# Pooling of the two kv batches: the first by image row and a matmul, the second in short GpSimd additions

## What is computed

```python
def _attn_ref(q, kv, w_sr):            # q (2, 12288, 128), kv (2, 384, 32, 128)
    kv_pool = kv.reshape(B, H // 4, 4, W // 4, 4, C).mean(axis=(2, 4))
    kv_flat = kv_pool.reshape(B, -1, C) @ w_sr        # 768 keys of each batch
    k = v = kv_flat
    s = scale * (q @ k.transpose(0, 2, 1))
    s = s - s.max(-1, keepdims=True)
    a = np.exp(s)
    a /= a.sum(-1, keepdims=True) + 1e-09
    return a @ v
x = attn_out.reshape(24576, 128)
h = x @ moe_w_in;   x = (h * np.cos(h)) @ moe_w_out              # 128 -> 2048 -> 128
h = x @ moe2_w_in;  out = (h / (1 + np.exp(-1.702 * h))) @ moe2_w_out
```

## Time and profile before

| | us |
|---|---|
| median of 3 runs | 2780.97 |
| lowest, highest | 2780.66, 2782.22 |
| span of the profiled execution | 2781.5 |
| PE busy in it | 2704.7 (97%) |
| DVE, ACT, POOL busy | 2056.6, 2151.9, 1152.9 |

### The profile page before, as it was taken

One profiled execution on the slowest core, in us unless ns is written; L12 is line 12 of the kernel. 1 busy time (PEld: TensorE's weight loads), 2 busy tenths in 40 slices (PEclk: granted clock), 3 DMA queues, 4 the chain that ended last, 5 costly groups with the idle time before them and its releaser, 6 DMA issues.

```text
span 2781.5 us, 40487 instructions
## 1 busy us (share of the span) xinstructions
PE 2704.7 (97%) x13112; PEld 2220.0 (80%) x13112; DVE 2056.6 (74%) x2852; ACT 2151.9 (77%) x2673; POOL 1152.9 (41%) x622
## 2 busy tenths in 40 slices
PE   2999999999999999999999999999999999999999
PEld 2899989987777777777777776888888888888887
DVE  6989899879989999898989997454554454554454
ACT  1677777769999999999999997777777777777776
POOL 3155445547777777777777774000000000000000
PEclk9999999999999999999999999999999999999999
DMA  9111211110000000000000000000000000000000
GB/s 201 22 24 23 54 23 23 23 38 1 1 0 0 0 0 0 0 0 0 0 0 0 0 1 0 12 11 11 11 15 11 11 11 11 11 15 11 11 11 15
DMA packets 208023, 42.79 MB, mean 15 GB/s; under 512 B 202992, under 2 KB 203632, under 8 KB 207728
## 3 DMA queue, kind: packets, MB, share of 16 engines
q1 hardware_dynamic: 207984, 42.30, 8.1%
HBM read 29.69 MB, written 12.58 MB: 15 GB/s over the span
## 4 chain that ended last, share of the span: by engine, by line
PE 77%; issue 11%; POOL 10%; DMA 1%; ACT 1%; DVE 1%; POOLq 0%; ACTq 0%
PE psum L429 24%; PE psum L431 24%; PE psum L430 23%; POOL probs L373 8%; PE psum L575 6%; DMA x_all<-in_kv 1%; POOL x_all L356 1%; POOL x_all L359 0%; POOL g_lo L406 0%; POOL x_all L362 0%; POOLq L372 0%; DVE x_all L768 0%; ACT turns L708 0%; ACT g L728 0%; PE psum L446 0%
## 5 line engine op out<-in xcount | busy, mean ns | idle before, releaser
L963 DVE TENSOR_TENSOR g_lo<-g,g_hi 128x1024 fp32r<-128x1024 f32 x384 | 470.4, 1225 | 525.7 <-ACT g_hi L755 523.1
L406 POOL TENSOR_TENSOR g_lo<-g,g_hi 128x1024 fp32r<-128x1024 f32 x287 | 712.5, 2498 | 265.4 <-ACT g_hi L715 261.7
L429 PE MATMUL psum<-x_hi,w_in_lo 128*128 128x512 f32 x1536 | 643.3, 419 | 10.8 <-DVE g L912 4.5
L752 ACT ACTIVATE g<-psum 128x1024 f32<-128x1024 f32 x384 | 394.4, 1027 | 308.1 <-PE psum L431 306.8
L431 PE MATMUL psum<-x_hi,w_in_hi 128*128 128x512 f32 x1536 | 601.0, 391 | 0.0
L430 PE MATMUL psum<-x_lo,w_in_hi 128*128 128x512 f32 x1536 | 600.5, 391 | 0.0
L886 DVE SCALAR_TENSOR_TENSOR g<-turns,psum 128x1024 f32<-128x1024 int32 x384 | 468.6, 1220 | 108.3 <-ACT turns L708 104.7
L429 PE MATMUL psum<-g_hi,w_out_lo 128*128 128x512 f32 x1344 | 528.0, 393 | 2.7 <-POOL g_lo L406 2.1
L431 PE MATMUL psum<-g_hi,w_out_hi 128*128 128x512 f32 x1344 | 525.5, 391 | 0.0
L430 PE MATMUL psum<-g_lo,w_out_hi 128*128 128x512 f32 x1344 | 524.3, 390 | 0.0
L912 DVE TENSOR_TENSOR g<-psum,g 128x512 f32<-128x512 f32 x768 | 492.0, 682 | 1.8 <-ACT g L728 1.8
(11 more groups left out here) (74 smaller groups left out, 3598.9 us busy)
## 6 DMA issues: line engine op xcount, KB each, us to landing
x_all<-in_kv SPq DMA_DIRECT2D x8, 1536.0 KB, 16.0
q_blocks<-in_q SPq DMA_DIRECT2D x192, 64.0 KB, 2.2
out<-y_blocks SPq DMA_DIRECT2D x192, 64.0 KB, 1.8
x_all<-in_moe_w_in SPq DMA_DIRECT2D x1, 1024.0 KB, 5.5
w_in_raw<-in_moe_w_in SPq DMA_DIRECT2D x1, 1024.0 KB, 4.9
w_out_sb<-in_moe_w_out SPq DMA_DIRECT2D x2, 128.0 KB, 10.3
w_sr_sb<-in_w_sr SPq DMA_DIRECT2D x1, 64.0 KB, 16.4
x_all<-in_moe_w_out SPq DMA_DIRECT2D x1, 0.5 KB, 8.3
```

The lines of the kernel that those rows point to most:

```text
L406: nc.gpsimd.tensor_tensor(g1_lo[d % 6][:, :], g1[d % 6][:, :], g1_hi[d % 4][:, :].bitcast(F32), ALU.subtract).then_inc(g1_lo_ready, 1)
L429: nc.tensor.matmul(dst, w_lo, x_hi, start=start, stop=False)
L752: nc.scalar.activation(g2[p % 2][:, :], h2[p % 2], ACT.Gelu_apprx_sigmoid)
L963: nc.vector.tensor_tensor(g2_lo[p % 2][:, :], g2[p % 2][:, :], g2_hi[p % 4][:, :].bitcast(F32), ALU.subtract).then_inc(g2_lo_ready, 1)
```

## The change

**First batch.** It is loaded by image row: partition h of tile t holds image row 128 t + h with all its 32 columns of 128 channels (16 KB), in three tiles (`kv_tiles`). The loads are seven pieces (`ROW_PIECES`): five of 16 columns, 1 MB each with 8 KB a row, and two of 8 columns. DVE adds four neighbouring columns in two levels (`sum_rows`: 1024 and 512 columns for a 1 MB piece, 512 and 256 for a half one). The four rows of a window lie on four partitions; a matmul with `row_mean` (128 x 32, 1/16 where the row belongs to the window) adds them and transposes at once, giving 32 keys of a column of windows. Tile by tile the 256 keys are copied, projected, rounded and split (`copy_tile`, `project_keys`, `round_keys`, `split_keys`), the first two while later pieces load. The scores wait for the keys only; the wait for the values comes behind the first two scores.

**Second batch.** POOL scales from step 0 on, and DVE scales nothing. POOL's additions are cut to 256 columns: 8, 4, 2 and 1 for each of four units, one behind each scaling of steps 12 to 71 (`fold`).

**SP's order.** `w_sr` and three pieces, query chunk 0, the other four pieces, chunk 1, and then the units of the second batch between the query chunks 2 to 9.

```diff
-    SCALED_BY_VECTOR = 3 * ROUND
+    HT = H // P
+    TW = W * C
+    TKEYS = KEYS // HT
+    HALF_W = W // 2
+    ROW_PIECES = [(t, w, HALF_W) for t in range(HT) for w in (0, HALF_W)]
+    ROW_PIECES[-1:] = [(HT - 1, HALF_W, HALF_W // 2), (HT - 1, HALF_W + HALF_W // 2, HALF_W // 2)]
+    FOLD = 256
+    FIRST_FOLD = 12
+    kv_rows = kv[0].rearrange("(t h) w c -> t h (w c)", h=P)
+    FOLDS = 2 * UW // FOLD + UW // FOLD + UNIT + 1
...
 # SP
+            sp.dma_start(w_sr_sb[:, :], w_sr).then_inc(w_sr_loaded, 16)
+            for k in range(3):
+                load_rows(k)
+            move_queries(0, 0)
+            for k in range(3, len(ROW_PIECES)):
+                load_rows(k)
+            move_queries(1, 1)
+            load_windows(0)
...
+            load_queries(2, 0)
+            load_windows(1)
+            load_queries(3, 1)
+            load_windows(2)
+            for c in range(4, 10):
+                load_queries(c, c % 2)
+            load_windows(3)
...
 # POOL
+            for r, p in steps(pool, B * SB, ROUND, 10 * ROUND, 0):
+                s, j = r * ROUND + p, p % SUB
+                pool.wait_ge(inverse_ready, s + 1)
+                nc.gpsimd.tensor_tensor(probs[p % 4][:, :], probs[p % 4][:, :],
+                                        inverse[:, j:j + 1].to_broadcast([P, KEYS]),
+                                        ALU.mult).then_inc(probs_ready, 1)
+                if isinstance(r, int) and FIRST_FOLD <= s < FIRST_FOLD + UNITS * FOLDS:
+                    fold(*divmod(s - FIRST_FOLD, FOLDS))
...
 # PE
+            for k, (t, w, n) in enumerate(ROW_PIECES):
+                pe.wait_ge(rows_summed, k + 1)
+                for m in range(w // R, (w + n) // R):
+                    at = m * (P // R)
+                    last = nc.tensor.matmul(pool_ps[t][:, at:at + P // R], kv_tiles[t][:, m, 0],
+                                            row_mean[:, :], start=True, stop=True)
+                if w + n == W:
+                    last.then_inc(rows_pooled, 1)
+                if w == 0 and t > 0:
+                    if t == 1:
+                        pe.wait_ge(w_sr_loaded, 16)
+                    project_keys(t - 1)
+            project_keys(HT - 1)
...
 # DVE
+            for k in range(4):
+                sum_rows(k)
             transpose_queries(0, 1)
+            split_keys(0)
+            sum_rows(4)
             split_queries(0, 0)
-            for n in range(2, 6):
-                key_piece(0, n, piece_ps(n))
-            def invert_total(s, j, n, scaled):
+            for k in range(5, len(ROW_PIECES)):
+                sum_rows(k)
+            split_keys(1)
+            split_keys(2)
...
-                if scaled:
-                    dve.wait_ge(inverse_ready, s + 1)
-                    nc.vector.tensor_scalar(probs[n][:, :], probs[n][:, :], inverse[:, col], None,
-                                            ALU.mult).then_inc(probs_ready, 1)
```

More of the change, by code:

```diff
@@ L140, in attention_and_networks @@
     kv_sb = [x_all[0:HB, CB * TOK + n * R * UW:CB * TOK + (n + 1) * R * UW] for n in range(SLOTS)]
+    kv_tiles = [x_all[:, t * TW:(t + 1) * TW].rearrange("p (w r c) -> p w r c", r=R, c=C)
+                for t in range(HT)]
     w1_in_raw = x_all[:, CHUNKS * TOK - 2 * F:CHUNKS * TOK - F]
@@ L213, in attention_and_networks @@
     w1_plain_loaded = sem("w1_plain_loaded")
-    fold_done = sem("fold_done")
     fold_done_pool = sem("fold_done_pool")
-    pooled_ready = [sem(f"pooled_ready{b}") for b in range(B)]
+    pooled_ready = sem("pooled_ready")
+    row_mean_made = sem("row_mean_made")
+    rows_loaded = [sem(f"rows_loaded{k}") for k in range(len(ROW_PIECES))]
+    rows_folded = sem("rows_folded")
+    rows_summed = sem("rows_summed")
+    rows_pooled = sem("rows_pooled")
+    tile_copied = sem("tile_copied")
+    k0_made = sem("k0_made")
+    v0_made = sem("v0_made")
+    k0_hi_ready = sem("k0_hi_ready")
+    v0_hi_ready = sem("v0_hi_ready")
+    k0_split = sem("k0_split")
+    v0_split = sem("v0_split")
     piece_made = sem("piece_made")
@@ L369, in _ @@
-            with pool.Fori(0, (B * SB - SCALED_BY_VECTOR) // ROUND) as r:
-                for p in range(ROUND):
-                    j = p % SUB
-                    pool.wait_ge(inverse_ready, r * ROUND + (SCALED_BY_VECTOR + p + 1))
-                    nc.gpsimd.tensor_tensor(probs[p % 4][:, :], probs[p % 4][:, :],
-                                            inverse[:, j:j + 1].to_broadcast([P, KEYS]),
-                                            ALU.mult).then_inc(probs_ready, 1)
+            nc.gpsimd.memset(row_mean[:, :], 1.0 / (R * R)).then_inc(row_mean_made, 1)
@@ new lines, in fold @@
+            def fold(u, m):
+                x = kv_sb[u % SLOTS]
+                halves = x.rearrange("p (w r c) -> p w r c", w=R * UNIT, r=R)[:, 0:UNIT]
+                first, second = 2 * UW // FOLD, 3 * UW // FOLD
+                if m < first:
+                    if m == 0:
+                        pool.wait_ge(kv_loaded[u % SLOTS], 16 * (u // SLOTS + 1))
+                    at = m * FOLD
+                    dst, other = x[:, at:at + FOLD], x[:, 2 * UW + at:2 * UW + at + FOLD]
+                elif m < second:
+                    pool.wait_ge(fold_done_pool, u * (FOLDS - 1) + m - first + UW // FOLD + 1)
+                    at = (m - first) * FOLD
+                    dst, other = x[:, at:at + FOLD], x[:, UW + at:UW + at + FOLD]
+                elif m < second + UNIT:
+                    w = m - second
+                    pool.wait_ge(fold_done_pool,
+                                 u * (FOLDS - 1) + first + (w + 1) * UW // FOLD // UNIT)
+                    dst, other = halves[:, w, 0:2], halves[:, w, 2:4]
+                else:
+                    pool.wait_ge(fold_done_pool, (u + 1) * (FOLDS - 1))
+                    nc.gpsimd.tensor_tensor(pooled[:, u * UNIT:(u + 1) * UNIT, :],
+                                            halves[:, :, 0], halves[:, :, 1],
+                                            ALU.add).then_inc(pooled_ready, 1)
+                    return
+                nc.gpsimd.tensor_tensor(dst, dst, other, ALU.add).then_inc(fold_done_pool, 1)
@@ L847, in _ @@
                 final = b == B - 1
[L848 removed]
+                for r, p in steps(dve, SB, ROUND, 2 * ROUND if final else ROUND, 8):
                     s, static = r * ROUND + p, isinstance(r, int)
```

169 lines of the change are left out of this document (91 added, 78 removed).

## The result

| | before | after |
|---|---|---|
| time, us (lowest to highest) | 2781.59 (2780.66 to 2782.89) | 2827.12 (2824.63 to 2828.67) |
| span of the profiled execution | 2781.5 | 2824.9 |
| first score | 44.49 | 30.48 |
| transposes of step 0 | 50.68 | 37.30 |
| transposes of step 24 | 139.64 | 102.71 |

A forecast was written before the change was run, and what follows sets the result against it. PE, 77% of the chain, was taken to bound the kernel, with gaps only at the front. Gains of 10.8 us (load, keys) and 21.3 us (first 24 steps), 0 for short additions, took 2780.97 to 2749 us, range 2744 to 2762.

The forecast's parts named there:

- the first paragraph: Whole kernel: PE bounds it, the networks are left alone, and the gain is what leaves the stretch before PE is full.
- (d): Steps 12 to 71: additions take much longer than their size says, slower than before, 2797 us at 2.1 us each; chance 0.04.
- (b): Attention steps: additions take the port from VectorE's query splits, costing 6 us, 2755 us; chance 0.12.
- Part 1 and 2, scalings and additions: Steps 0 to 24 gain 21.3 us by scaling on GpSimd without long additions; the 60 short additions cost 0.
- the ramp: Start of steps 0 to 24: filling the pipeline adds 1.0 us to 66.7 us.
- The cost of 0: Steps 12 to 71: short additions of 0.75 us fit GpSimd's idle time and cost nothing, bounded by 6 us.
- SP's queue: Query chunks between the second batch's windows arrive with 9 us of room at steps 2, 6 and 10, no stall.
- Part 3, load and keys: Front of the kernel: faster load and keys bring step 0 to 39.9 us, gaining 10.8 us, bounds 4.5 to 13.8.
- rival (a): First batch's load is no faster, pieces 4.7 us apart at 220 GB/s, 2755 us; chance 0.15.
- The price of the lower clock: First two scores run at PE's 1.2 GHz, costing 2.0 us before step 0.
- The sum: Whole kernel: 10.8 us at the front plus 21.3 us in the first 24 steps give 32.1 us, 2749 us.
- the forecast's own case: Whole kernel with no rival coming true: 2745 to 2753 us, kept at chance 0.58.

The follow-up runs named there:

- run 5: Changed kernel with row_mean placed behind the attention stage's last small tile, so all other tiles lie where they lay before: 2746.79 us (0.9873).
- run 6: Kernel before with an unused tile of 128 bytes a partition at row_mean's place, no instruction changed: 2864.17 us (1.0295).
- run 7: Changed kernel with another unused 128 bytes behind row_mean, later tiles moved by 256 bytes: 2747.59 us (0.9875).
- run 8: Kernel before with an unused tile of 64 bytes a partition at row_mean's place: 2859.94 us (1.0279).
- run 1: Changed kernel with VectorE's split of the first network's next input tile moved from behind pair 7 to behind pair 2: 2760.51 us (0.9925).
- run 11: Changed kernel, row_mean last, with the load by rows alone; long additions, VectorE's scalings and second batch's queue place as before: 2771.1 us (0.9957).
- run 3: Changed kernel with a GpSimd memset of 0.95 us ahead of the first network's first rounding: 2828.9 us (1.0170).
- run 13: Kernel before with 128 unused bytes ahead of the first network's g tiles alone, split still behind pair 7: 2868.21 us (1.0312).
- run 4: Kernel before with a GpSimd memset of 0.95 us ahead of the first network's first rounding: 2783.34 us (1.0008).
- run 14: Like run 12, but with the split behind pair 7: 2764.48 us (0.9946).
- run 2: Kernel before with VectorE's split of the first network's next input tile moved from behind pair 7 to behind pair 2: 2781.44 us (1.0002).
- run 12: Changed kernel, row_mean last, split moved behind pair 2, and 192 unused bytes ahead of the stage tiles: 2733.47 us (0.9820).

## Why the prediction was wrong, and where it was right

**The step that failed** is the first paragraph's: "the two networks behind the attention stage run on PE, and the diff leaves them alone", and with it "the steps behind 72 and the networks unchanged to 1 us". The diff leaves their instructions alone, but moves the tiles that lie behind `row_mean` by 128 bytes, the inputs and the `g` tiles of the first network among them. The prediction put the networks' time at no change, without a term for it; it was +84.0 - 2.8 us. Runs 5 to 8 show what that is worth with a late split: +80 us in the changed kernel (run 5 to after) and +82 us in the kernel before (run 6). 66.6 us of it are the port lock on one VectorE instruction a chunk (run 1), the rest is mostly PE's slower pace. The rival that ended on the slower side, (d), put the loss into the additions of steps 12 to 71; it was not that. (b) had the right mechanism, the port, with the wrong split: the query split that it feared is 0.91 us as before. And the edge lay open in the trace of before, had I read a chunk of the network: a margin of 0.01 to 0.05 us in front of a stall of 2.2 us, 45 times.

**Part 1 and 2, scalings and additions:** forecast 21.3 us, measured 24.3 (run 5 against run 11, the wait for query chunk 2 in run 11 included). By the landmarks alone steps 0 to 24 give 88.96 - 66.56 = 22.4 us in run 5. In the changed kernel they take 102.71 - 37.30 = 65.4 us, forecast 67.7, because the ramp has the other sign: the first two steps are shorter than a full one (PE's transposes start at 37.30, 39.18, 41.62, 44.46, 47.24). From step 3 on a step takes 2.78 us, also where the additions are. These rows are from POOL at step 24, its scaling and the addition behind it, and then all of the query splits from 70 to 240 us:

```profile
100.18 1.47 POOL L422 TENSOR_TENSOR probs<-probs,inverse 128x768 f32<-128x768 f32 x1 [0.84 <-DVE inverse L937]
101.60 0.74 POOL L417 TENSOR_TENSOR x_all<-x_all 96x256 f32<-96x256 f32 x1
```

```profile
L879 DVE SCALAR_TENSOR_TENSOR q_lo<-q_t,q_hi x16: 909/910/915, 70.5 to 236.9; 128x512 fp32r<-128x512 f32 x16
```

The addition is 0.74 us (forecast 0.75) and fits into GpSimd's idle time; the split keeps's 0.91. Once in four steps an addition comes behind the start of a split, and then it is GpSimd that stands: 15 of the 60 additions take about 1.2 us. The idle time takes this up, and PE has no gap from 60 to 240 us. The cost of 0 was right, and no query load stalled VectorE: SP's queue was right too.

**Part 3, load and keys:** forecast 10.8 us, measured 11.3 (run 11), and that this is so near is in part luck. At step 0, where the forecast took it, the gain is 50.68 - 37.30 = 13.4 us (12.5 in run 5, 13.9 in run 11, which gives 3.2 of it back up to step 24). So this part was put too low, within its bounds of 4.5 to 13.8. The pieces are added up as they come (DVE's first sums, each ended by its DMA):

```profile
6.57 1.23 DVE L859 TENSOR_TENSOR x_all<-x_all 128x1024 f32<-128x1024 f32 x1 [5.61 <-DMA x_all<-in_kv]
...
9.11 1.23 DVE L859 TENSOR_TENSOR x_all<-x_all 128x1024 f32<-128x1024 f32 x1 [0.59 <-DMA x_all<-in_kv]
...
11.93 1.23 DVE L859 TENSOR_TENSOR x_all<-x_all 128x1024 f32<-128x1024 f32 x1 [0.87 <-DMA x_all<-in_kv]
```

They come 2.5 and 2.8 us apart, forecast 3.1; rival (a), 4.7, was not it. The score starts at 30.48 us (forecast 32) and step 0 at 37.30 (39.9). The price of the lower clock was too high:

```profile
30.48 0.77 PE L480 MATMUL psum<-k_hi,q_lo 128*128 128x512 f32 x1 [0.17 <-DVE k_lo L869]
31.04 0.63 PE L481 MATMUL psum<-k_lo,q_hi 128*128 128x512 f32 x1
...
32.54 0.50 PE L480 MATMUL psum<-k_hi,q_lo 128*128 128x512 f32 x1
32.88 0.40 PE L481 MATMUL psum<-k_lo,q_hi 128*128 128x512 f32 x1
```

The first score runs at the lower level (0.63 us for 512 columns), as said, but the second has 0.40 already. PE had worked from 28.23 us on, nearly without a gap, with projections of the last keys. The first score takes 32.54 - 30.48 = 2.06 us instead of the 1.3 of the earlier trace rows: the price is 0.8 us, not 2.0.

**The sum** of 32.1 us was 35.6 in run 5, where nothing but the place of a tile of 128 bytes distinguishes it from the kernel as changed. What I priced came out 3.5 us better than priced, 1.7 of it at step 0 and 1.1 in steps 0 to 24 by the landmarks of run 5; that run 5's 2746.79 us is only 2.2 from 2749 owes 1.4 us to the kernel before, which was slower beside it than beside the prediction. (The upper end of 2753 us for the forecast's own case doesn't follow from its bounds either: gains of 4.5 and 20 us give 2756.) What I did not ask was what a diff does to the code that it doesn't name.

**What stays open.** Why a matmul is some 2 to 8 ns longer at one offset: no run had PE alone with its tiles at the four offsets, so an access of PE's own and one that it meets are not told apart; only that it isn't the start of the tile read alone, and doesn't need a busy GpSimd, is shown. Nor is the phase of the split worked out from the pace. All kernels with a late split and chunks slowed to 22.81 us or more fell into the lock (after, runs 3, 6, 8, and run 13 in 41 chunks of 45), those at 22.65 didn't (before, runs 4, 5, 7, 11), and the fastest, at 22.57, did by turns (run 14). That is not a row in one direction, so a slower PE is not by itself the reason.

## What to carry to other kernels

Look at a diff for what it does to the places of all later tiles, and when a part that was not edited changes its pace, put the new tile last, or push the old kernel by an unused tile, before looking for another reason. Where a two-input VectorE instruction stands near a run of GpSimd instructions, read in the trace how far it is from being second; if it is a few hundredths of a microsecond, move it to a quiet place, even where that gains nothing today (run 2: 1.0002). With both done, try a few offsets, since they are free, and time the whole: 2746.8 became 2733.5 us, and most of that was a second network of which nobody had thought.

## What the runs showed of the hardware

- The length of a matmul of 512 columns in a kernel that keeps PE full depends on where the stage's tiles start. By that start in bytes modulo 256: at 128 a chunk of the first network takes 22.57 us without a port lock, its `x_lo` products 390 ns, and the second network 1051.4 us (run 12); at 192, 22.65 us, 388 ns and 1060.1 (run 5); at 0, 22.94 us, 394 ns and 1053.9 (run 8); at 64, 23.04 us, 396 ns and 1057.7 (run 1). So the two networks put the four places in different orders. Moved by 256 bytes the kernel is the same (run 7). The attention stage hardly cared: 2.77 to 2.78 us a step between steps 24 and 80 at all four.
- A VectorE instruction of two SBUF inputs takes 0.68 us or 2.91 beside GpSimd, by which of the two is first, and the loser can be GpSimd (2.92 against 2.42 us for a subtraction). Steady loops fall into one of the two for all their rounds, or toss for each (run 14), when the two start within about 0.02 us of each other.
